# A wider inverse table in the last stage of a long convolution: sums of 128 columns in place of 98

## What is computed

```python
def _attn_ref(x, v, pos_emb, w1, w2):
    ...
    u = x * v
    L = 2 * S
    Uf = np.fft.rfft(u, n=L, axis=1)
    Hf = np.fft.rfft(h_filt, n=L, axis=0)
    y = np.fft.irfft(Uf * Hf[None, :, :], n=L, axis=1)[:, :S, :]
    return (x * y).astype(np.float32)

def reference(...):
    attn_out = _attn_ref(...)
    x = _moe_ref(x=attn_out, ...)      # relu(x @ w_in)**2 @ w_out
    return _moe2_ref(x=x, ...)         # g @ w_out, g = h for h > 0, alpha * h below
```

## Time and profile before

| | us |
|---|---|
| median of 3 runs | 1447.92 |
| lowest and highest | 1447.65, 1450.24 |
| profiled execution | 1447.91 |
| its span, first to last instruction | 1446.1 |
| PE busy in it | 1426.0 |

### The profile page before, as it was taken

How to read it: one execution, slowest core, us unless ns; L and a number is a source line. 1 busy time by engine, 2 the same in 40 slices (tenths; PEclk the granted TensorE clock), 3 DMA queues, 4 the chain that set the end, 5 groups by cost and what they waited for, 6 DMA issues and landing times.

```text
span 1446.1 us, 20433 instructions
## 1 busy us (share of the span) xinstructions
PE 1426.0 (99%) x6996; PEld 1247.7 (86%) x6996; DVE 1116.6 (77%) x1389; ACT 1142.1 (79%) x1553; POOL 69.1 (5%) x60
## 2 busy tenths in 40 slices
PE   8999999999999999999999999999999999999996
PEld 8998888898888888888888888888888888888885
DVE  6876666546877788777888888888888888888885
ACT  3676677446887788877888888888888888888885
POOL 4510011211000000000000000000000000000000
PEclk9999999999999999999999999999999999999999
DMA  8545877442011101100000000000000000000000
GB/s 256 179 145 169 296 227 271 142 138 68 1 30 30 30 1 30 29 7 8 7 7 7 0 7 7 7 7 7 7 5 1 7 7 7 7 7 7 1 7 14
DMA packets 47014, 79.14 MB, mean 55 GB/s; under 512 B 4697, under 2 KB 29503, under 8 KB 46191
## 3 DMA queue, kind: packets, MB, share of 16 engines
q1 hardware_dynamic: 44622, 68.43, 15.2%
q10 hardware_dynamic: 2208, 9.97, 2.0%
q0 software_dynamic: 128, 0.02, 0.0%
HBM read 59.10 MB, written 19.23 MB: 54 GB/s over the span
## 4 chain that ended last, share of the span: by engine, by line
PE 97%; DVE 1%; ACT 1%; issue 0%; DMA 0%; SPq 0%; DVEq 0%; ACTq 0%
PE ps L152 13%; PE ps L164 12%; PE ps L166 12%; PE ps L165 12%; PE ps L153 12%; PE ps L151 12%; PE ps L663 6%; PE ps L629 4%; PE ps L725 4%; PE ps L644 3%; PE ps L652 3%; PE ps L637 1%; PE ps L612 1%; DVE stage L343 1%; DVE g_lo L355 0%
## 5 line engine op out<-in xcount | busy, mean ns | idle before, releaser
L355 DVE TENSOR_TENSOR g_lo<-stage,g_hi 128x960 fp32r<-128x960 f32 x207 | 239.4, 1157 | 155.9 <-ACT g_hi L268 155.9
L164 PE MATMUL ps<-g_hi,w_hi 128*128 128x480 f32 x832 | 318.7, 383 | 9.6 <-DVE g_lo L355 8.3
L152 PE MATMUL ps<-x_hi,w_lo 128*128 128x480 f32 x832 | 318.4, 383 | 0.0
L166 PE MATMUL ps<-g_lo,w_hi 128*128 128x480 f32 x832 | 317.8, 382 | 0.0
L165 PE MATMUL ps<-g_hi,w_lo 128*128 128x480 f32 x832 | 316.3, 380 | 0.0
L151 PE MATMUL ps<-x_hi,w_hi 128*128 128x480 f32 x832 | 315.7, 379 | 0.0
L153 PE MATMUL ps<-x_lo,w_hi 128*128 128x480 f32 x832 | 314.5, 378 | 0.0
L305 ACT ACTIVATE stage<-ps,sign_sb 128x480 f32<-128x480 f32 x416 | 252.4, 660 | 70.3 <-PE ps L153 66.1
L343 DVE SCALAR_TENSOR_TENSOR stage<-stage,alpha_sb 128x480 f32<-128x480 f32 x416 | 279.5, 713 | 24.2 <-ACT stage L305 23.9
L384 DVE TENSOR_TENSOR g_lo<-g,g_hi 128x960 fp32r<-128x960 f32 x208 | 240.0, 1154 | 13.6 <-ACT g_hi L294 13.6
L277 ACT ACTIVATE relu<-ps 128x960 f32<-128x960 f32 x208 | 203.1, 976 | 54.3 <-PE ps L153 48.8
(11 more groups left out here) (54 smaller groups left out, 1171.5 us busy)
## 6 DMA issues: line engine op xcount, KB each, us to landing
work<-dft_back SPq DMA_DIRECT2D x49, 256.0 KB, 3.0
g_dram<-work SPq DMA_DIRECT2D x49, 256.0 KB, 3.4
gt<-g_dram SPq DMA_DIRECT2D x12, 784.0 KB
gt<-x_seq SPq DMA_DIRECT2D x32, 196.0 KB
work<-v_seq SPq DMA_DIRECT2D x32, 196.0 KB
work<-dft_forward SPq DMA_DIRECT2D x49, 128.0 KB, 3.3
x<-x_gate ACTq DMA_DIRECT2D x4, 1560.0 KB, 8.0
out_t<-x SPq DMA_DIRECT2D x26, 240.0 KB, 2.0
```

The costliest lines, as they stand in the source:

```text
L152: nc.tensor.matmul(into[:, c, :T], w_lo[k][:, at], x_hi[layer][:], start=False, stop=False)
L164: nc.tensor.matmul(acc[layer][:, :T], w_hi[k][:, at], hi[:, c], start=first, stop=False)
L166: last = nc.tensor.matmul(acc[layer][:, :T], w_hi[k][:, at], lo[:, c], start=False, stop=end)
L355: nc.vector.tensor_tensor(g_lo[1][:, at], g2[at], g_hi[1][:, at].bitcast(FP32), ALU.subtract).then_inc(g2_lo_ready, 1)
```

## The change

The table gets 30 columns of zeros behind its 98, so that it is 98 x 2 x 128. Each matmul of the last stage streams 128 columns and gives a sum of 128 columns of which the last 30 are zero. In `sum_half` the four sums lie at column 128 times n and fill the 512 columns of a bank. The gate reads the first 98 (or 97) of each, as before. Number and order of the instructions stay; the buffers that are allocated behind the table lie 240 bytes further on in each partition.

```diff
@@ sums() in sum_first_group
-                last = nc.tensor.matmul(ps[:, bank, :R], gt_buffers[0][:R, half, n, blk * P:(blk + 1) * P],
+                last = nc.tensor.matmul(ps[:, bank, :P], gt_buffers[0][:R, half, n, blk * P:(blk + 1) * P],
                                         idft98_sb[:R, half], start=half == 0, stop=half == 1)
@@ sum_half
-                last = nc.tensor.matmul(ps[:, 6 + blk, R * n:R * (n + 1)],
+                last = nc.tensor.matmul(ps[:, 6 + blk, P * n:P * (n + 1)],
                                         gt_buffers[b][:R, half, n, blk * P:(blk + 1) * P], idft98_sb[:R, half],
                                         start=half == 0, stop=half == 1)
@@ gate_half
-            y = ps[:, 6 + h % 2, :GN * R].rearrange("p (n m) -> p m n", m=R)[:, :rows, :]
+            y = ps[:, 6 + h % 2, :].rearrange("p (n m) -> p m n", m=P)[:, :rows, :]
@@ shape_constants
-    idft98 = np.stack([g.real, -g.imag], 1).reshape(2, R, R).transpose(1, 0, 2)
+    idft98 = np.zeros((R, 2, P))
+    idft98[:, :, :R] = np.stack([g.real, -g.imag], 1).reshape(2, R, R).transpose(1, 0, 2)
@@ build
-        idft98_sb = sb("idft98_sb", [P, 2, R])
+        idft98_sb = sb("idft98_sb", [P, 2, P])
```

## The result

| | before | changed |
|---|---|---|
| median of 12 executions each | 1448.15 us | 1444.55 us |
| lowest and highest | 1446.21, 1450.24 | 1442.31, 1446.78 |
| changed / before | | 0.9976, 95% interval 0.9968 to 0.9984 |
| profiled execution, its span | 1447.91, 1446.1 | 1445.81, 1444.0 |

The change is 0.24% faster, 0.75 us above the forecast 1443.8 and inside its range. The profiled execution is one of the slower ones of the changed kernel, 1.3 us above its median.

What follows compares the result with a forecast made beforehand. The prediction took TensorE to bound the kernel, busy 1426.0 of 1446.1 us. From 1447.9 us it took off 4.1 (5.1 from the clock less 1.0 of DMA wait), giving 1443.8 us, range 1441.8 to 1448.3.

Steps and rivals of the forecast that it cites:

- Pace of the records: Last stage's 512 records: 30 more columns hidden by the next weight load, 0 taken of 0 to +1.0 us.
- Rival D: Last-stage records: streaming not covered by weight loads, up to 12.8 us slower, 1460.7 us; chance 0.06.
- That the gain comes by the clock: Around 284 us: wider records keep TensorE's granted clock up, giving back 5.1 us before any new wait.
- forecast A: Around 284 us: the clock stays up, 1443.8 us, own range 1441.2 to 1446.6; chance 0.53.
- A's sign for the pace: Profile of L725: durations still 275 ns and 16 records in 1.76 us.
- its signs around 284: Clock 1.00 in 285 to 290, 32 records in 3.5 us, first long product at 287.6, idle up to 2 us.
- B: Clock still falls at 284 but returns in under 4 us, by 288: gain 3.4 us, 1444.5; chance 0.16.
- four stretches: Kernel start, 284.1 to 290.7, 278 to 284, and drain: clock returned or held with wide records, not with 98 columns.
- The price of a low clock: From 284.08 to 298.86: 14.78 us in the chain, 9.67 at full clock, a gain of 5.1 us.
- The wait for the third group: TensorE, asking at 288.9 us, waits for the third group's 784 KB load: 1.0 us taken of 0 to 2.8.
- net gain: Last stage around 284 us: 5.1 us from the clock less 1.0 us of DMA wait, 4.1 us.
- Costed at nothing: Wider table's load, the gate's reads at pitch 128, unread zero sums, buffers 240 bytes on: 0, allowing a few tenths.

Runs made afterwards that it cites:

- e8_narrow: Kernel before with the wide table's layout, half groups streaming 64 columns (sums of rows 64 to 97 left out), first group 98: 1452.48 us, 1.0040 of before.
- e1_layout: Changed kernel's wide table, moved buffers and PSUM pitch of 128, but every last-stage matmul streams 98 columns: 1448.37 us, 1.0000 of before.
- e5_gap: Kernel before (98 columns) with five useless float32 matmuls filling TensorE's idle before 282 us: 1448.46 us, 0.9998 of before.
- e2: Changed kernel's layout, only the first group's 32 records streaming 128 columns, half groups 98: 1447.28 us, 0.9995 of before.
- e4: Changed kernel using all 128 array rows in the last stage, the table having 30 rows of zeros too: 1445.15 us, 0.9980 of before.
- e9: Changed kernel with the third group's load split, its first 98 rows loaded in step 36 of the loop: 1444.36 us, 0.9969 of before.
- e12: Changed kernel with the third group's load split and early, and useless records filling the idle before 282 us: 1442.32 us, 0.9958 of before.
- e7: Changed kernel with useless work filling the idle before 282 us and the drain's first idle: 1444.29 us, 0.9977 of before.
- e6: Kernel before (98 columns) with useless work filling the idle before 282 us and the drain's first idle: 1448.35 us, 0.9993 of before.
- e3: Changed kernel's layout, only the half groups' 480 records streaming 128 columns, first group 98: 1445.96 us, 0.9988 of before.
- e10: Kernel before (98 columns) with the third group's load split, its first 98 rows loaded in step 36: 1448.07 us, 1.0000 of before.

## Why the prediction was right, point by point

**Pace of the records: right.** 0 was taken of 0 to 1.0 us; the half groups are 4.40 us apart in place of 4.39, that is 0.01 x 30 = 0.3 us at most. The row of L637, the same shape elsewhere in the kernel, was the right one to take. Rival D is out. That the next weight load hides the columns is likely but not shown; e8_narrow shows only that 64 to 128 columns cost the same. The Trainium skill, page "TensorE: Matmul & The Clock Gate", section "Back-to-back issue gap", would by its isolated formula have had these records get slower with their columns. Its other sentence, that in a stream of pairs of load and matmul both operations set the spacing, fits the trace better: 110 ns per record with 98 columns, 112 at most with 128.

**That the gain comes by the clock: right, and shown.** Streaming alone brings it (e1_layout has the layout without it and gains nothing), less streaming costs 0.40% (e8_narrow), the lower level lasts 3.4 us or more longer with 98 columns at the same place (five traces of 98 against three of 128), and filling the idle of the kernel before with useless work gives 1442.82 us in the execution that kept its clock (e5_gap).

**How it comes: forecast A is half of it, and the near hit is partly luck.** A had the clock stay up at 284. The changed kernel's own profile shows A's sign for the pace (16 records in 1.79 us) and none of its signs around 284: its clock fell at 284, the 32 records took 6.94 us and the first long product came at 290.85. It came back after 6.8 us, which is B in kind, though B had it back by 288. The profiles of e2, e4 and e9 show A's picture, and 6 of the 12 executions have at most one short stretch, which fits A with the drain's fall. So the median of 1444.55 is that of a mixture of both, and that it lies 0.75 us from A's price is not A's doing alone. I had taken the start of the kernel, with L612's records, as B's measure; the same number of columns on 98 rows took longer. What was missing in the forecast is that where the clock falls against the work is not fixed: I read four stretches of one execution as if they were every execution. One of the four I also read wrongly: the products of 480 columns that begin at 290.80 end at 293.3, where the third group begins, so the clock rose at 294.3 a us into 98-column records again and not 3.5 us into long products.

**The price of a low clock: right, 0.3 us too high.** 5.1 us were forecast for the stretch at full clock; 14.67 - 9.83 = 4.8 us were measured (e12).

**The wait for the third group: right place, too small.** In the stretch it costs 11.66 - 9.83 = 1.8 us in e2 where 1.0 was taken, so the net gain is 3.0 us and not 4.1; the idles are 1.57 and 1.35 us in e2 and e4, 2.64 and 2.70 in e5 and e7, and 0 to 2.8 was the bound. The reason given, that the two loads run nearly one behind the other, does not hold: in e2 PE could begin 6.2 us after the load's issue (284.77 to 290.96) near the 6.7 us of both together; in e5 it was 5.0 us, half way between those and the 3.3 of one alone. By medians of whole executions the price comes to 3.3 us: 1447.8 at 0.995 before, 1444.52 at 0.999 after. What the forecast did not see is that this wait is itself an idle in which the clock can fall, or just behind it (e5, e6, e7).

**Costed at nothing: right.** Table, pitch, PSUM reads and the shift of 240 bytes: 1.0000 with its interval of 0.0009 (e1_layout).

**Sums.** Two small slips change nothing: both loads together, 6.7 us from 284.67, are through at 291.4 and not 291.7, and the share within 0.2% adds up to 0.34, not 0.35.

**Left open:** why the last store landed after 4.6 and 4.5 us in the profiled executions of e5 and e7 and not in others; and what exactly of a matmul the gate sees. The runs say that more columns in the same time help, and do not say how much rows count.

## What to carry to other kernels

Here moving columns were free up to 128, the length of the weight load (256 cost twice as much, 216 ns per record against 110), and zeros in them were worth having: with them TensorE keeps its clock around an idle more often, and gets it back sooner. Look at the mean granted clock of every execution, not at one profile: a low stretch of 3 to 10 us that comes in some executions is both the noise and the gain of such a change. Before counting the gain of a stretch that gets faster, ask which transfer it then waits for, and whether that wait costs the clock again.

## What the runs showed of the hardware

- With an idle of 1.8 us between the first group's float32 records of 98 columns the clock fell in each of the five profiles (before, e1, e3, e8, e10), and 77 of 86 executions have a mean of 0.995 or less, over 13 us at the lower level. With 128 columns on both sides it fell in one profile of three (changed; not e4, e9), and none of 12 executions has 0.995 or less.
- Once low, the clock stayed low through 6.6 us of unbroken 98-column records, and through 6.7 us of unbroken 128-column records on 98 rows, at the end of which it rose (changed kernel, 284.1 to 290.8).
- At 64 moving columns a dense run of 48 records lost the clock with no idle over 0.23 us (331 us in e8_narrow).
- The last 256 KB store of the loop landed 2.4 us after its issue before and 4.6 us after it in e5, and two loads of 784 KB issued 0.4 us apart let PE go on 6.2 us after the first one's issue (e2).
- A float32 record with a load of 128 columns has a pace of 108 to 112 ns for 64, 98 and 128 moving columns at 2.4 GHz, and 211 ns at 1.2 GHz for 98 and 128 alike (32 records from 284.03 to 290.80 in the earlier trace rows, from 284.09 to 290.85 after).
